# Second-batch keys split on ACT and Pool instead of DVE, the gates' product in another PSUM bank, and three copies in another order

## The reference

```python
scores = scale * np.matmul(q, k.transpose(0, 1, 3, 2))        # batch 2, 8 heads, 576 x 576, head size 64
kth = np.partition(scores, -top_k, axis=-1)[..., -top_k:-top_k + 1]
scores = np.where(scores >= kth, scores, -1000000000.0)
attn = softmax(scores); x = attn @ v                          # 1152 tokens x 512
h = x @ w_in; g = np.maximum(h, 0.0) + alpha * np.minimum(h, 0.0); x = g @ w_out
logits = x @ w_gate; noise_scale = np.log1p(np.exp(x @ w_noise))
noisy_logits = logits + noise_scale * noise                   # the two best experts of each token
out += top2_w * (np.maximum(x @ w1[e], 0.0) @ w2[e])
```

## Time and profile before

| | before |
|---|---|
| median of three runs | 817.15 us (816.07 to 817.48) |
| the profiled execution | 817.79 us |
| its span (first to last instruction) | 816.0 us |
| PE busy | 692.6 us, 85% of the span |
| DVE, ACT, POOL busy | 543.6, 449.2, 371.9 us |
| PE waits for ACT's copy of the gates | 9.9 us in 6 waits |
| PE waits for ACT's copy of x^T | 8.0 us in 6 waits |
| PE waits for ACT's copy of the scores | 18.7 us in 12 waits |

### The profile page before, as it was taken

One profiled execution on the slowest core, in us unless ns is written; L12 is line 12 of the kernel. 1 busy time (PEld: TensorE's weight loads), 2 busy tenths in 40 slices (PEclk: granted clock), 3 DMA queues, 4 the chain that ended last, 5 costly groups with the idle time before them and its releaser, 6 DMA issues.

```text
span 816.0 us, 13507 instructions
## 1 busy us (share of the span) xinstructions
PE 692.6 (85%) x4516; PEld 538.7 (66%) x4516; DVE 543.6 (67%) x1163; ACT 449.2 (55%) x814; POOL 371.9 (46%) x421
## 2 busy tenths in 40 slices
PE   2553899988888999999998989726999999999993
PEld 2443566755555666666766656525899899899893
DVE  6997998987776869789787612572555555545520
ACT  6765666756555756666675543551445445445421
POOL 3655976764446676676675651360022022022022
PEclk9967999999989999999999999976999999999998
DMA  9394013005101504040260044237083583484422
GB/s 308 133 373 180 14 53 141 29 2 200 56 16 43 170 3 156 14 142 26 77 206 0 1 148 162 88 146 270 1 268 102 172 270 114 156 270 127 145 33 33
DMA packets 36720, 98.89 MB, mean 121 GB/s; under 512 B 10480, under 2 KB 11504, under 8 KB 35184
## 3 DMA queue, kind: packets, MB, share of 16 engines
q1 hardware_dynamic: 32288, 88.31, 31.1%
q0 software_dynamic: 4384, 9.98, 5.5%
HBM read 80.15 MB, written 37.34 MB: 144 GB/s over the span
## 4 chain that ended last, share of the span: by engine, by line
PE 74%; DVE 9%; ACT 7%; issue 4%; DMA 2%; POOL 2%; SPq 0%; ACTq 0%; DVEq 0%; POOLq 0%
PE bank L892 15%; PE bank L923 13%; PE bank L1072 11%; PE ps_scores L1058 9%; PE bank L872 6%; PE bank L1058 5%; PE bank L1077 4%; DVE top L381 4%; DVE rest L387 3%; PE bank L856 3%; PE ps_scores L819 3%; ACT scores L1140 2%; PE bank L904 2%; PE bank L1040 1%; DMA k_raw<-kt_in_dram 1%
## 5 line engine op out<-in xcount | busy, mean ns | idle before, releaser
L381 DVE MAX8 top<-rest 128x8 f32<-128x576 f32 x216 | 152.3, 746 | 0.0
L1486 POOL TENSOR_TENSOR expo<-scores,expo 128x576 f32<-128x576 f32 x72 | 101.6, 1412 | 107.0 <-ACT scores L1140 106.9
L892 PE MATMUL bank<-w_in_sb,x_t 128*128 128x512 f32 x272 | 131.1, 627 | 17.9 <-ACT gate L1250 9.9
L1603 POOL DMA_INDIRECT out_dram<-ye,xe x24 | 42.8, 1784 | 217.2 <-ACT ye L1395 212.4
L923 PE MATMUL bank<-w_out_high,g_parts 128*128 128x512 f32 x288 | 101.9, 415 | 4.8 <-DVE g_parts L578 4.8
L387 DVE MATCH_REPLACE8 rest<-top,rest 128x576 f32<-128x576 f32 x144 | 105.7, 741 | 0.0
L892 PEld LDWEIGHTS bank<-w_in_sb,x_t 128*128 128x128 f32 x272 | 52.6, 202 | 73.6 <-issue 64.5
L1072 PE MATMUL bank<-w_hi,he_t 128*128 128x512 f32 x256 | 91.9, 400 | 0.0
L585 DVE TENSOR_TENSOR w_lo<-raw,w_hi 128x1024 fp32r<-128x1024 f32 x64 | 77.9, 1225 | 19.4 <-ACT w_hi L1338 18.5
L381 DVE MAX8 top<-scores 128x8 f32<-128x576 f32 x72 | 53.2, 753 | 53.8 <-ACT scores L1109 32.2
L819 PE MATMUL ps_scores<-k_parts,q_high 128*128 128x288 f32 x160 | 56.4, 365 | 29.2 <-ACT scores L1109 18.7
(11 more groups left out here) (189 smaller groups left out, 1522.3 us busy)
## 6 DMA issues: line engine op xcount, KB each, us to landing
raw<-w_dram SPq DMA_DIRECT2D x64, 512.0 KB, 9.6
x_sorted_dram<-x_sorted_dram SPq DMA_DIRECT2D x7, 2570.0 KB, 10.4
q_raw<-q_rows_dram SPq DMA_DIRECT2D x18, 256.0 KB, 2.6
xe<-x_sorted_dram SPq DMA_DIRECT2D x8, 514.0 KB, 4.5
w_out_raw<-w_out_dram SPq DMA_DIRECT2D x4, 1024.0 KB, 13.0
w_in_sb<-w_in_dram SPq DMA_DIRECT2D x4, 1024.0 KB, 8.8
out_dram<-x_now SPq DMA_DIRECT2D x1, 3584.0 KB, 27.7
x_sorted_dram<-x_now SPq DMA_DIRECT2D x1, 2570.0 KB, 18.9
```

Source lines behind the costliest of these rows:

```text
L381: nc.vector.max(dst, src).then_inc(chain if r < ROUNDS - 1 else dve_top, 1)
L892: mm = pe.matmul(dst, x_t[:, k, :], w_in_sb[:, k, c * 512:(c + 1) * 512], start=(k == 0), stop=(k == MK - 1))
L1486: nc.gpsimd.tensor_tensor(expo[:, n % 4, :], scores[:, n % SBUFS, :], expo[:, n % 4, :], ALU.mult).then_inc(pool_prob, 1)
```

## The change

- The low halves of batch 1's keys leave DVE. For each head ACT now casts the lower half into `k_high`, then rounds the upper half, and POOL subtracts (`low_keys(1, head)`). There is one scratch, so ACT's cast for head h waits until POOL has subtracted head h - 1. `K_HIGH_AT` and `K_HIGH_BEHIND` give ACT's tiles (ahead of `copy_scores`, and behind `copy_other`), `K_LOW_AT` POOL's.
- The gates' product goes to columns 256 to 271 of `ps_pt4`. The wait for `act_gate` leaves the first layer and stands before the transposes at h = 0. `copy_gates` stands before the signs.
- `copy_x_t` stands right behind `copy_prob_t`, before signs and scores.
- The row sums of block 0's second half stand after the second pair of block 1 (before: after the first).
- Other scores stand behind the first layer (odd h) or behind the values product (even h).
- SP: `blank_rows(2)` goes ahead of the second half of block 4's queries, and `second_values(2)` ahead of the second half of block 5's.

```diff
-K_HIGH_AT = {24: (0,), 25: (1,), 29: (2,), 30: (3, 4), 31: (5, 6), 32: (7,)}
-K_LOW_AFTER = {12: (0, 1), 15: (2, 3), 16: (4, 5), 17: (6, 7)}
+K_HIGH_AT = {22: 0, 24: 1, 29: 2, 30: 4, 31: 6}
+K_HIGH_BEHIND = {29: 3, 30: 5, 31: 7}
+K_LOW_AT = {24: (0,), 26: (1,), 30: (2,), 31: (3, 4), 32: (5, 6), 33: (7,)}
...
+        loop_gates = ps_pt4[:, 2 * P:2 * P + 2 * EXPERTS]
...
-                    if isinstance(blk, int) and PAIRS * blk + pair in K_LOW_AFTER:
-                        second_low_keys(PAIRS * blk + pair)
...
-                    if pair == (0 if second else 1) and not first:
+                    if pair == 1 and not first:
                         row_sums(blk - 1, 1)
...
-            next_queries(MIXED)
+            next_queries(MIXED, [0])
             blank_rows(2)
+            next_queries(MIXED, [1])
...
                 wait(pe, act_pt, tile)
+                if h == 0:
+                    wait(pe, act_gate, blk - 2)
...
                     wait(pe, act_h1, 4 * j + c)
-                    if c == CHUNKS - 1:
-                        wait(pe, act_gate, j)
...
-                    if isinstance(tile, int) and tile in OTHER_AT:
-                        other_scores(OTHER_AT[tile])
                     if h % 2 == 0 or h == 1:
                         prob_values(tile, h, blk, mixed_block, b)
                     if mlp and h in FIRST_AT:
                         first_layer(blk - 1, FIRST_AT[h])
+                    if isinstance(tile, int) and tile in OTHER_AT:
+                        other_scores(OTHER_AT[tile])
...
                 act.wait_ge(k_in_second[h // 2], 16)
                 at = k_slot(1, h)
+                act.wait_ge(k_low, HEADS + h)
+                nc.scalar.copy(k_high, k_raw[DIM:, at, :].rearrange("p (a b) -> p a b", b=DIM)).then_inc(act_k_high, 1)
                 nc.scalar.copy(k_parts[0:DIM, at, :], k_raw[0:DIM, at, :]).then_inc(act_k, 1)
...
                     copy_prob_t(tile, h)
+                    if mlp and h == 1:
+                        copy_x_t(blk - 1)
+                    if rest and h == 7:
+                        copy_gates(blk - 2)
...
+                    if isinstance(tile, int) and tile in K_HIGH_AT:
+                        second_high_keys(K_HIGH_AT[tile])
                     if not (last and h + AHEAD >= HEADS):
                         copy_scores(tile + AHEAD, h + AHEAD)
...
+                    if isinstance(blk, int) and HEADS * blk + h in K_LOW_AT:
+                        pool.wait_ge(pool_prob, HEADS * blk + h + 1)
+                        for head in K_LOW_AT[HEADS * blk + h]:
+                            low_keys(1, head)
```

More of the change, by code:

```diff
@@ L400, in row_sums, with one_block @@
                 nc.vector.reciprocal(rden[:, half, :], den[:, half, :]).then_inc(dve_rden, 1)
[L402 to L416, removed]
+            def one_block(blk, first=False, mixed=False, after_mixed=False):
                 for pair in range(PAIRS):
                     topk_pair(HEADS * blk + 2 * pair, 2 * pair, PAIRS * blk + pair, mixed)
-                    if isinstance(blk, int) and PAIRS * blk + pair in K_LOW_AFTER:
-                        second_low_keys(PAIRS * blk + pair)
                     if pair == 1 and after_mixed:
                         row_sums(blk - 1, 0)
-                    if pair == (0 if second else 1) and not first:
+                    if pair == 1 and not first:
                         row_sums(blk - 1, 1)
@@ L456, in _ @@
             one_block(0, True)
-            one_block(1, second=True)
+            one_block(1)
             one_block(2)
@@ L849, in other_scores, with prob_transpose @@
                 score_parts(i, b, head).then_inc(pe_other, 1)
-            def prob_transpose(tile, h):
+            def prob_transpose(tile, h, blk):
                 pe.wait_ge(pool_prob, tile + 1)
                 wait(pe, act_pt, tile)
+                if h == 0:
+                    wait(pe, act_gate, blk - 2)
                 for kt in range(KT):
@@ L934, in x2_transpose, with gates @@
                 mm.then_inc(pe_x2t, 1)
-            def gates(j, chunks, dst=ps_h, src=xf.rearrange("p (k n) -> p k n", k=MK)):
+            def gates(j, dst=loop_gates, src=xf.rearrange("p (k n) -> p k n", k=MK)):
                 pe.wait_ge(act_x2t, j + 1)
-                pe.wait_ge(act_h1, chunks)
+                wait(pe, act_gate, j)
                 for k in range(MK):
-                    mm = pe.matmul(dst[:, 0:2 * EXPERTS], src[:, k, :], gates_w[:, k, :],
+                    mm = pe.matmul(dst, src[:, k, :], gates_w[:, k, :],
                                    start=(k == 0), stop=(k == MK - 1))
@@ L948, in one_block @@
                     tile = HEADS * blk + h
-                    prob_transpose(tile, h)
+                    prob_transpose(tile, h, blk)
                     if not (last and h + AHEAD >= HEADS):
@@ L973, in one_block @@
                     if rest and h == 6:
-                        gates(blk - 2, 4 * blk - 1)
+                        gates(blk - 2)
             def rank(turn, bank):
@@ L1014, in _ @@
             first_layer(j, 3, last_h[3], alone=True)
-            gates(j - 1, 4 * j, ps_pt4, x2_t.rearrange("p (k n) -> p k n", k=MK))
+            gates(j - 1, ps_pt4[:, 0:2 * EXPERTS], x2_t.rearrange("p (k n) -> p k n", k=MK))
             for c in range(CHUNKS):
@@ L1027, in _ @@
             x2_transpose(j, ps_t, chunks=4 * j + 4)
-            pe.wait_ge(act_gate, j)
-            gates(j, 4 * j + 4, src=x_t)
+            pe.wait_ge(act_h1, 4 * j + 4)
+            gates(j, ps_h[:, 0:2 * EXPERTS], src=x_t)
             pe.wait_ge(act_relu, 4 * BLOCKS)
@@ L1264, in one_block @@
                         copy_x2_t(blk - 2, xf, ps_y)
-                    if rest and h == 7:
-                        copy_gates(blk - 2)
                     if not last and h in Q_HIGH_AT:
@@ L1287, in one_block @@
                         copy_other(OTHER_AT[tile])
-                    for head in K_HIGH_AT.get(tile, ()) if isinstance(tile, int) else ():
-                        second_high_keys(head)
+                    if isinstance(tile, int) and tile in K_HIGH_BEHIND:
+                        second_high_keys(K_HIGH_BEHIND[tile])
                     if h % 4 == 3:
@@ L1354, in _ @@
             copy_x2_t(j - 1, x2_t, ps_pt)
-            copy_gates(j - 1, ps_pt4)
+            copy_gates(j - 1, ps_pt4[:, 0:2 * EXPERTS])
             gap_exp(0, EARLY, 0)
@@ L1471, in _ @@
             for h in range(2, HEADS):
-                low_keys(h)
+                low_keys(0, h)
                 if h == 3:
```

22 lines of the change are left out of this document (10 added, 12 removed).

## The result

| | before | after |
|---|---|---|
| median | 817.27 us (816.07 to 817.48) | 783.76 us (782.21 to 784.89) |
| ratio, 95% interval | | 0.9592 [0.9571, 0.9612] |
| profiled execution, span | 817.79, 816.0 us | 783.08, 781.3 us |

The kernel is 33.5 us faster by the medians and 34.7 by the spans.

What follows compares the result with a forecast made beforehand. DVE sets the pace in tiles 8 to 16, PE in blocks 5 and 6, idling 3.2 to 3.5 us a block. 4.5 + 7.5 + 9.9 + 3.0 + 4.5 = 29.4 us off 817.79 gives 788.4, median 788, range 779 to 797.

Steps and rivals of the forecast that it cites:

- Row sums, 4.5: Block 1: DVE no longer waits 4.53 us for ACT's output copy, its chain comes earlier; 4.5 us gained, least 3.0.
- x^T, 7.5: First layer: six waits for x^T, 8.0 us, go, some 0.5 returns at tile 25; 7.5 us gained, bounds 4 and 8.
- Gates, 9.9: First layer's last chunk: six waits for the gates' copy go, the moved wait is hidden; 9.9 us gained, bounds 8 and 9.9.
- Keys and other scores, 3.0: Tiles 27 to 34: waits of 14.4 us fall to 10.6, about 0.8 more gained at tile 33; 3.0 us less.
- Stalls 2.5: Tile 30: ACT, before casting head 4, waits 2.5 us for POOL to subtract head 3.
- 2.7 us later: Tile 31: with heads 5 and 6, ACT's scores copy comes 2.7 us after PE's first layer ends.
- The clock, 4.5: PE's half clock after idle time: 3.0 us back behind gate waits, 1.6 in tiles 27 to 34; 4.5 taken, bounds 0 and 8.
- DMAs, nothing: Loads on SP: blank rows issued at tile 22 instead of 26 and the reordered queries neither gain nor cost time.
- Handed back: Rival: new waits of 1 us a block, no clock gain, chain at its upper bound; about 800 us, chance 0.17.
- Nothing: Rival: DVE's pairs really pace the blocks, PE's waits are their shadow; within 0.2% of before, chance 0.02.
- The ping-pong: Rival, ACT at tiles 29 to 31: casts of heads 3 to 7 each wait a whole DVE pair; 836 us, chance 0.03.
- The chain doesn't bind: Rival: POOL reaches head 3 before ACT needs the scratch; 8 us more and fewer clock drops, 779 us, chance 0.15.

Runs made afterwards that it cites:

- the run with the late copy: Changed kernel with the copies of the gates behind the signs again, the gates' own bank kept: 785.32 us, ratio 0.9613.
- the kernels with the chain loosened: Changed kernel with POOL subtracting heads 3 and 5 one tile earlier: 777.91 us; with ACT's casts also behind its scores copy: 777.00 us.

## Why the prediction held, step by step

It said 788 (779 to 797), and 783.76 came out: by its own sum 29.4 us were forecast and 34.0 came up to tile 71. The causes that it named are the ones that the traces show; one of its sizes, the row sums', came out near by luck, as said below.

- **Row sums, 4.5.** 4.97 in tiles 9 and 12, so not the bound of 3.0. But 4.97 isn't 4.5 by the mechanism given. The row sums left the front of the pair together with the wait of 4.53, and they are 0.74 + 0.18 us more: POOL's thresholds begin at 73.29 in place of 79.35, that is 6.06 earlier, 5.80 when counted from the start of tile 8. PE's idle time in tile 9 fell by 5.56 and its wait ahead of tile 13 by 0.46; the slow clock took 1.04 back in tile 9. Seven other kernels have both this edit and that of x^T; from tile 8 to the end of tile 17 they take 56.8 to 57.5 us, after 56.35 and before 64.36, so after's profiled execution is the luckiest of the eight. Where the others save at tile 13 they can lose it at tile 17: two with the full clock at tile 13 wait 1.67 and 1.65 us there for POOL's x. "The row sums (0.74 us ...)" was too dear for their new place: the first of them takes 0.13 us when nothing stands beside it. In the earlier trace rows it began at 67.28 beside POOL's probabilities (66.59 to 68.00 in that trace), and ended with them at 68.02. After has the same again, in tile 32:

```profile
220.53 1.23 DVE L399 TENSOR_TENSOR den<-o_sb,least 128x4 f32<-128x4 f32 x1 [4.84 <-ACT o_sb L1162]
```

```profile
220.33 1.41 POOL L1477 TENSOR_TENSOR expo<-scores,expo 128x576 f32<-128x576 f32 x1
```

  It ends at 221.76, 0.02 us behind POOL's end at 221.74. The Trainium skill (SBUF — State Buffer, Who interferes with whom) says that a DVE instruction with two SBUF inputs and a POOL instruction that reads SBUF exclude each other; this row agrees (1.23 us, median of the 18 is 0.154). What the prediction feared by that rule, that POOL's key subtractions hold up DVE's small one, doesn't show: DVE's four small subtractions in tiles 27 to 34 took 0.15 to 0.16 us. POOL's own 14 took 1.312 to 1.329 us. DVE idles 63.77 - 39.74 = 24.0 us in that stretch, so a delay of its own would have cost nothing there.
- **x^T, 7.5.** 5 x 1.40 + 0.24 = 7.24. Each wait was worth 1.40 and not the 1.33 of its bracket. Tile 25 kept 1.16 us of it, not "some 0.5". The late copy on ACT is the 0.5 foreseen; beside it PE waits for x, which POOL makes behind a key subtraction of tile 24 that the prediction left out here:

```profile
165.23 0.65 PE L870 MATMUL bank<-ident,x 128*128 128x128 f32 x4 [0.36 <-POOL x L1490]
...
166.40 0.95 PE L861 MATMUL bank<-v,prob_t 128*64 128x65 f32 x20 [0.51 <-ACT prob_t L1148]
```

- **Gates, 9.9.** 2.02 a tile, 0.23 more than the bracket of 1.79, at five tiles: 10.1. The copy's earlier place, given as one of two covers, isn't needed (the run with the late copy). The Trainium skill's rule on guarding by bank (PSUM — Partial Sum Buffer, PSUM bank collisions raise a hardware error) only moved the wait, and the moved wait is nothing, as said.
- **Keys and other scores, 3.0.** Idle time fell 4.84. "Stalls 2.5" and "2.7 us later" are the steps that held best: the stall is 2.65, PE's waits are 4.69 (4.6) and 2.87 (2.7), and POOL's chain is 10.33 (10.2). The size was off by 1.84: tile 32's wait is 0.39 and not the 1.6 put down, and the 0.8 of other idle time at tile 33 (14.4 - 10.6 - 0.8 = 3.0 is its sum) didn't come. That "by that alone 14.4 would fall to about 3" held too: 3.31 with the keys on DVE. What the prediction didn't say is that its own two figures, about 3 and 10.6, make the keys' move the one part that loses time. The runs put its price at 9 to 11 us, 6.25 of it idle time in tiles 27 to 34.
- **The clock, 4.5.** 3.0 came behind the gates' waits (as said), 1.6 in tiles 29 to 32 (1.6 said), and 1.65 at tile 13, which the prediction overlooked: 6.2 in all. The 1.04 that the slow clock took back in tile 9 was overlooked too. That the slow clock goes where a wait goes isn't sure: it left tiles 23 and 63 with x^T alone as well, with the gates' waits still there. The sum was short by 4.6 us: 1.7 of clock, 0.6 of busy time beside the waits, 1.84 of idle time in tiles 27 to 34, 0.5 of row sums (tile 9's clock in it) and 0.2 of gates, less 0.3 of x^T.
- **DMAs, nothing.** Right, and shown in both kernels.
- **The rivals.** "Handed back" fell: the two plain blocks take 46.1 and 45.9 us and no new wait shows in them. "Nothing" fell with it. The ping-pong stayed two stalls of 2.6 us. "The chain doesn't bind" is what the kernels with the chain loosened show, at 777 to 778. That this is close to its 779 is chance: loosening gave 6 to 7 us against after and not the 8 put down. The terms of "handed back" (29.4 - 6 - 4.5 - 3.5) lead to 802 and not to 800.

## What to carry to other kernels

Before work is moved from a busy engine to idle ones, ask whether the busy one sets the pace there: DVE didn't, and the move put a single scratch between two engines, in front of a copy that the pace-setter waits for. When two waits of one engine lie close together, the list of waits names only the first, so the second comes up when the first goes. Look at each part of a change alone and at the whole with each part undone; a gain of 4% hid a part that cost 1.1 to 1.3%.

## What was not expected of the hardware

The granted clock of PE fell to 1.2 of 2.4 GHz behind the same wait in one kernel and not in another, with the same work around it. The clearest case is the last chunk of the first layer at tile 23, behind 1.79 us of waiting for the gates. It took 5.14 us in the kernel before and 3.67 with x^T alone moved:

```profile
162.86 3.67 PE L892 MATMUL bank<-w_in_sb,x_t 128*128 128x512 f32 x8 [1.79 <-ACT gate L1250]
```

At tile 63 behind the same 1.79 us it took 5.17 us before, 5.37 with the row sums alone and 3.67 with x^T, the other scores or the keys alone.

At tile 13 the length of the wait goes with the outcome, but not wholly. The clock fell behind all seven waits of 2.64 to 3.19 us, and stayed full behind six of the seven waits of 2.55 to 2.58. The exception is the kernel with DVE's keys and the old loads (wait 2.57). Here is its tile 13, then that of the kernel with the new loads (wait 2.58):

```profile
95.95:103.19 7.24, 7.24 (x37) 3.79 (x37) 7.19 (x16) 3.51 (x7) 6.84 (x9) 0.76 0.00 0
```

```profile
97.17:102.72 5.55, 5.55 (x38) 3.22 (x38) 5.55 (x13) 3.48 (x7) 5.15 (x8) 1.00 0.00 0
```

So 1.5 to 1.7 us a time hang on something other than the wait's length, and the time of a kernel is uncertain by a few of these. In the 27 executions of the kernel before, the mean granted clock is 0.935 and 0.937 in the two slowest (820.7 and 820.9 us) and 0.950 and 0.953 in the two fastest (810.1 and 812.0). What else decides it, these runs don't show.

A wait also costs 0.07 to 0.23 us more than its bracket: tiles shortened by 1.40 and 2.02 us where 1.33 and 1.79 stood. At tile 27, at the full clock before and after, 2.49 us went with a bracket of 2.27, and the other 0.22 had counted as busy time of PE (6.24, now 6.02).
